# Two feed-forward layers behind an attention kernel: widening products by Strassen's algorithm in sets of seven, narrowing products in blocks behind them

## The reference

```python
scores = np.where(q_bucket == k_bucket, scale * q @ k.T, -1e9)
x = softmax(scores) @ v               # regrouped to x: 1536 x 512
h = sigmoid(x @ w_gate) * (x @ w_val) # widening, 512 -> 1536
x = h @ w_out                         # narrowing, 1536 -> 512
h = x @ w_in                          # widening, 512 -> 2048
g = where(h >= 1, h, where(h <= -1, 0, (h + 1)**2 / 4))
out = g @ w_out2                      # narrowing, 2048 -> 512
```

## Time and profile before

| | us |
|---|---|
| median of 3 runs | 810.24 (810.23 to 810.4) |
| the profiled execution | 812.36 |
| its span, first to last instruction | 810.3 |
| TensorE (PE) busy | 798.3 |
| its weight loads (PEld) | 687.4 |
| VectorE (DVE) busy | 377.4 |
| ScalarE (ACT) busy | 393.3 |
| GpSimd (POOL) busy | 241.6 |

### The profile page before, as it was taken

One profiled execution on the slowest core, in us unless ns is written; L12 is line 12 of the kernel. 1 busy time (PEld: TensorE's weight loads), 2 busy tenths in 40 slices (PEclk: granted clock), 3 DMA queues, 4 the chain that ended last, 5 costly groups with the idle time before them and its releaser, 6 DMA issues.

```text
span 810.3 us, 10651 instructions
## 1 busy us (share of the span) xinstructions
PE 798.3 (99%) x4015; PEld 687.4 (85%) x4015; DVE 377.4 (47%) x624; ACT 393.3 (49%) x636; POOL 241.6 (30%) x248
## 2 busy tenths in 40 slices
PE   7999999999999999999999999999999999999997
PEld 7899999999888888888888888888888888888886
DVE  5888888888793211131112221234434443344333
ACT  4889988988995332121112232335434333343332
POOL 4567767866865633000000043422100000000000
PEclk9999999999999999999999999999999999999999
DMA  6896586465302331000000023220000100010001
GB/s 140 175 204 139 125 171 140 89 138 122 101 1 74 122 114 55 1 1 1 0 1 1 0 78 105 79 78 27 1 0 1 53 1 0 1 53 0 1 1 52
DMA packets 62002, 49.51 MB, mean 61 GB/s; under 512 B 28592, under 2 KB 51840, under 8 KB 61824
## 3 DMA queue, kind: packets, MB, share of 16 engines
q1 hardware_dynamic: 61792, 48.83, 25.0%
q10 hardware_dynamic: 160, 0.00, 0.0%
HBM read 27.27 MB, written 3.15 MB: 38 GB/s over the span
## 4 chain that ended last, share of the span: by engine, by line
PE 90%; DVE 4%; ACT 3%; issue 2%; DMA 1%; POOL 0%; SPq 0%; ACTq 0%
PE ps L569 17%; PE ps L571 17%; PE ps L570 17%; PE ps L545 6%; PE ps L693 5%; PE ps L695 5%; PE ps L694 5%; PE ps L562 3%; PE ps L563 3%; PE ps L533 3%; PE ps L536 3%; DVE probs L952 2%; PE ps L496 2%; DVE body L963 1%; ACT body L733 1%
## 5 line engine op out<-in xcount | busy, mean ns | idle before, releaser
L569 PE MATMUL ps<-xh,arena 128*128 128x512 f32 x480 | 186.9, 389 | 0.0
L571 PE MATMUL ps<-xh,arena 128*128 128x512 f32 x480 | 186.8, 389 | 0.0
L570 PE MATMUL ps<-xl,arena 128*128 128x512 f32 x480 | 186.8, 389 | 0.0
L425 POOL TENSOR_TENSOR arena<-stage,arena 128x1024 fp32r<-128x1024 f32 (+1 forms) x26 | 73.4, 2831 | 253.5 <-ACT arena L763 253.5
L1022 DVE TENSOR_TENSOR gate<-ps,gate 128x512 f32<-128x512 f32 x36 | 24.9, 692 | 200.6 <-ACT gate L821 200.6
L821 ACT ACTIVATE gate<-ps 128x512 f32<-128x512 f32 x36 | 21.5, 598 | 176.9 <-PE ps L571 176.9
L963 DVE TENSOR_TENSOR body<-ps,body 128x768 fp32r<-128x768 f32 x96 | 91.7, 956 | 32.4 <-ACT body L733 31.2
L569 PEld LDWEIGHTS ps<-xh,arena 128*128 128x128 f32 x480 | 90.1, 188 | 18.9 <-issue 0.4
L571 PEld LDWEIGHTS ps<-xh,arena 128*128 128x128 f32 x480 | 90.1, 188 | 18.8
L570 PEld LDWEIGHTS ps<-xl,arena 128*128 128x128 f32 x480 | 90.1, 188 | 18.6
L418 POOL TENSOR_SCALAR probs<-probs,small 128x768 f32<-128x768 f32 x96 | 86.8, 913 | 25.5 <-DVE small L957 22.7
(11 more groups left out here) (95 smaller groups left out, 1194.0 us busy)
## 6 DMA issues: line engine op xcount, KB each, us to landing
stage<-in_moe_w_out_dram SPq DMA_DIRECT2D x28, 256.0 KB, 3.3
body<-qh SPq DMA_DIRECT2D x15, 384.0 KB, 5.3
body<-kh SPq DMA_DIRECT2D x28, 192.0 KB, 5.4
stage<-in_moe_w_in_dram SPq DMA_DIRECT2D x16, 256.0 KB, 2.8
qn<-in_q_dram SPq DMA_DIRECT2D x16, 192.0 KB, 4.6
kn<-in_k_dram SPq DMA_DIRECT2D x16, 192.0 KB, 5.8
body<-ql SPq DMA_DIRECT2D x16, 192.0 KB, 5.7
vn<-in_v_dram SPq DMA_DIRECT2D x16, 192.0 KB, 2.6
```

What stands on the lines that cost most here:

```text
L569: pe.matmul(dst, wh, ah, start=start, stop=False)
L570: pe.matmul(dst, wh, al, start=False, stop=False)
L571: return pe.matmul(dst, wl, ah, start=False, stop=stop)
```

## The change

The hidden features are now made in sets. A set takes 256 features (F) for one batch of 768 tokens, contraction 512, as a product of 2 x 2 blocks, and makes it with Strassen's algorithm (the form with 15 additions) from seven products instead of eight, each with 256 of contraction, 128 features and 384 tokens. There are 24 sets for the first layer (N1; gate and value in turns, six pairs for each batch) and 16 for the second (N2, "hinge"). FIRSTS are the sets 0, 12, 24, 32, where a new batch or layer begins.

The sums of the weight blocks (four of 256 elements a set) are made on POOL, as are the low parts (low_a: 512 and 256 elements, low_s: 1024), after ScalarE's round_w; only two sets of split weights are kept, and each batch makes them again. The four sums of the x blocks and the seven low parts are made on VectorE, 768 elements each (sum_x, rest_x), the high parts on ScalarE (round_x); for set 0 four sums are on POOL within the last attention steps. Products use PSUM banks 6 and 7 in turn (4 and 5 in sets 0 and 1). ScalarE copies out the first product of a set, VectorE adds the others to what it has (empty). In the first layer the value's set ends in gate_quarter (384 elements) and gate_tiles (768 and 384). A hidden tile is 128 features x 768 tokens; round_tile (ScalarE) and rest_tile (VectorE) split it. empty_y copies a finished narrowing result out of PSUM. In the narrowing of the first layer each block of 128 output features takes 768 tokens as 512 and 256 columns. Behind the seventh product of each set stands a block of narrowing work of earlier tiles (units, down): four units of six matmuls in the first layer, eight in set 24, twelve of three matmuls in the others. hinge_part is Relu and Square of 768 elements on ScalarE.

```diff
+    R = 7
+    F = 2 * P
+    N1, N2 = 2 * B * (T1 // 2), B * (T2 // 2)
+    NSETS = N1 + N2
+    FIRSTS = (0, N1 // 2, N1, N1 + N2 // 2)
+    PAIRS1 = N1 // 2
+    TILES1 = 2 * PAIRS1
...
+        LEFT = (0, 4, 1, 5, 3, 2, 6)
+        def bank(n, r):
+            q = R * n + r
+            return ps[:, (4 if n < 2 else 6) + q % 2, 0:G]
+        def emptied(n, r):
+            if r < 0:
+                n, r = n - 1, r + R
+            return (e_dve, (R - 1) * n + r) if r else (e_act, n + 1)
...
+            for n in range(2, NSETS):
+                sp.wait_ge(w_split, 2 * (n - 1))
+                load_w(n)
+                if 2 < n < N1 // 2 and n % 2:
+                    sp.wait_ge(wo_split, n // 2)
+                    load_wo(wo_v, n // 2)
+                if N1 <= n < FIRSTS[3]:
+                    sp.wait_ge(wo_split, T1 // 2 + n - N1)
+                    load_wo(wo2_v, n - N1)
...
-            def product(dst, wh, wl, ah, al, start, stop):
-                pe.matmul(dst, wh, ah, start=start, stop=False)
-                pe.matmul(dst, wh, al, start=False, stop=False)
-                return pe.matmul(dst, wl, ah, start=False, stop=stop)
-            def up1(g, f, which):
-                pe.wait_ge(w_split, f + 1)
-                if not (g == 0 and f < 2):
-                    pe.wait_ge(gated, T1 * g + f - 1)
-                for m in which:
-                    dst = ps[:, 4 + 2 * m + f % 2, :]
-                    for c in range(KT):
-                        if f == 0 and m == 0:
-                            pe.wait_ge(xh_ready, 2 * g + c // 2 + 1)
-                            pe.wait_ge(xl_ready, 2 * g + c // 2 + 1)
-                        at_w = 2 * C1 * f + DM * m + P * c
-                        last = product(dst, arena[:, at_w:at_w + P], arena[:, at_w + C1:at_w + C1 + P],
-                                       xh[:, c, :], xl[:, c, :], c == 0, c == KT - 1)
-                if 1 in which:
-                    last.then_inc(hid_ready, 1)
+            def product(n, r):
+                if r < 2:
+                    pe.wait_ge(w_split, 2 * n + r + 1)
+                if n in FIRSTS:
+                    pe.wait_ge(x_low, low_count(group_of(n), r))
+                if n == 2 and r == 0:
+                    pe.wait_ge(o_last, 3)
+                if R * n + r > 1:
+                    pe.wait_ge(*emptied(n, r - 2))
+                high, low = weights(n, 0)[:, LEFT[r]], weights(n, 1)[:, LEFT[r]]
+                dst = bank(n, r)
+                for c in range(2):
+                    pe.matmul(dst, high[:, c, :], high_x(r)[:, c, :], start=(c == 0), stop=False)
+                    pe.matmul(dst, high[:, c, :], low_x(r)[:, c, :], start=False, stop=False)
+                    last = pe.matmul(dst, low[:, c, :], high_x(r)[:, c, :], start=False, stop=(c == 1))
+                last.then_inc(p_done, 1)
...
+            def down1(t, c):
+                if c == 0:
+                    tile_waits(t)
+                wh, wl = narrow(t)
+                cols, first, last_tile = slice(P * c, P * c + P), t % T1 == 0, t % T1 == T1 - 1
+                main, rest = ps[:, c, :], ps[:, 4 + c // 2, (S - 512) * (c % 2):(S - 512) * (c % 2) + S - 512]
+                if first and c % 2 == 0:
+                    pe.wait_ge(zeroed, 1)
+                    pe.matmul(ps[:, 4 + c // 2, :].rearrange("p (a n) -> p a n", a=2), zero[:, :],
+                              hh[:, t % 3, 512:S].rearrange("p (a n) -> p a n", a=1).to_broadcast([P, 2, S - 512]),
+                              start=True, stop=False)
+                for n, (w, h) in enumerate(((wh, hh), (wh, hl), (wl, hh))):
+                    pe.matmul(main, w[:, cols], h[:, t % 3, 0:512], start=(first and n == 0), stop=(last_tile and n == 2))
+                    last = pe.matmul(rest, w[:, cols], h[:, t % 3, 512:S], start=False,
+                                     stop=(last_tile and n == 2 and c % 2 == 1))
...
+            def units(n, r):
+                if n < 2 or r < R - 1:
+                    return 0
+                return KT if n < N1 else 2 * KT if n == N1 else 2 * T
...
             pe.wait_ge(ends[held[2][0]], held[2][1] + 1)
-            up1(0, 0, (0,))
+            product(0, 0)
+            product(0, 1)
             turn_probs(STEPS - 3)
             turn_probs(STEPS - 2)
             for part in range(HT):
                 weigh(2 * NH - 2, part)
             turn_probs(STEPS - 1)
-            up1(0, 1, (0,))
+            product(0, 2)
+            product(0, 3)
             for part in range(HT):
                 weigh(2 * NH - 1, part)
-            pe.wait_ge(o_last, 2)
-            up1(0, 0, (1,))
-            pe.wait_ge(o_last, 3)
-            up1(0, 1, (1,))
+            for r in range(4, R):
+                product(0, r)
+            for n in range(1, NSETS):
+                for r in range(R):
+                    product(n, r)
+                    for _ in range(units(n, r)):
+                        down()
+            last2 = TILES1 + 2 * T2 - 2
+            for r in range(T):
+                down2(last2, r)
+            for r in range(T):
+                down2(last2 + 1, r)
...
+            def first_product(n):
+                act.wait_ge(p_done, R * n + 1)
+                if n:
+                    act.wait_ge(*emptied(n - 1, 2))
+                    if widens(n - 1) == "value":
+                        act.wait_ge(half_gated, pair_of(n - 1) + 1)
+                act.copy(u1[:, :], bank(n, 0)).then_inc(e_act, 1)
+            def sigmoids(n):
+                pp = pair_of(n)
+                for second in (1, 0):
+                    act.wait_ge(*emptied(n, 6 - second))
+                    act.activation(hidden(pp, second), hidden(pp, second), ACT.Sigmoid).then_inc(sig_done, 1)
...
+            def gate_set(n):
+                pp, after = pair_of(n), n in FIRSTS
+                g = group_of(n)
+                if n == FIRSTS[1] + 2:
+                    empty_y(0)
+                first_product(n)
+                round_tile(2 * pp - 2)
+                if after:
+                    round_x(g, 5)
+                    round_x(g, 6)
+                round_tile(2 * pp - 1)
+                round_w(n + 1)
+                sigmoids(n)
...
+            def hinge_set(n):
+                pp, g = pair_of(n), group_of(n)
+                t = 2 * pp
+                ahead = n + 1 in FIRSTS
+                first_product(n)
+                round_tile(t - 2)
+                if n in FIRSTS:
+                    round_x(g, 5)
+                    round_x(g, 6)
+                if t - 1 > TILES1:
+                    hinge_part(t - 1)
+                if ahead:
+                    round_x(g + 1, 0)
+                    round_x(g + 1, 1)
+                round_tile(t - 1)
+                if n + 1 < NSETS:
+                    round_w(n + 1)
+                if n < FIRSTS[3]:
+                    f = n - N1
+                    if f < T1 // 2:
+                        act.wait_ge(tile_used, TILES1 // 2 + 2 * f + 2)
+                    else:
+                        act.wait_ge(x_low, 3 * R)
+                    round_wo(T1 // 2 + f, (narrow2(2 * f), narrow2(2 * f + 1)))
+                if ahead:
+                    round_x(g + 1, 2)
+                    round_x(g + 1, 3)
+                hinge_part(t)
+                if ahead:
+                    round_x(g + 1, 4)
+                if n in (N1, FIRSTS[3]):
+                    empty_y(g - 1)
...
+            def empty(n, r):
+                pp = pair_of(n)
+                value = widens(n) == "value"
+                dve.wait_ge(p_done, R * n + r + 1)
+                one, two = hidden(pp, 0), tmp if value else hidden(pp, 1)
+                if r == 1:
+                    dve.wait_ge(*emptied(n, 0))
+                    if n:
+                        dve.wait_ge(*emptied(n - 1, 6))
+                        if widens(n - 1) == "value":
+                            dve.wait_ge(gated, 2 * pair_of(n - 1) + 2)
+                    dst, other = u2, u1
+                elif r == 2:
+                    if pp > 1 and not value:
+                        dve.wait_ge(hl_ready, 2 * (pp - 1))
+                    dst, other = u1 if value else one[:, 0:G], u1
+                elif r == 3:
+                    dve.wait_ge(*emptied(n, 1))
+                    dst, other = u3, u2
+                elif r == 4:
+                    dve.wait_ge(*emptied(n, 3))
+                    dve.tensor_tensor(two[:, G:S], bank(n, 4), u3, ALU.add)
+                    dst, other = u2, u2
+                elif r == 5:
+                    dst, other = two[:, 0:G], u3
+                else:
+                    dve.wait_ge(*emptied(n, 4))
+                    dst, other = u2 if value else one[:, G:S], u2
+                dve.tensor_tensor(dst, bank(n, r), other, ALU.add).then_inc(e_dve, 1)
+            def rest_tile(t):
+                dve.wait_ge(hh_ready, t + 1)
```

(102 more changed lines are left out.)

728 lines of the change are left out of this document (396 added, 332 removed).

## The result

The changed kernel takes 867.29 us (median of four runs) against 810.32 for the kernel before on the same chip: ratio 1.0707, 95% interval 1.0686 to 1.0728. The prediction had the direction, and VectorE as the engine that TensorE waits for, but its range ended at 866 (the bounds that it worked out itself went to 871). The profiled execution took 867.23 us for a span of 865.1; the forecast's sum, made against the span of before, was 810.3 + 32.8 = 843.1, so 22 us more than forecast are to be found, beside the 33 that were forecast.

A forecast was written before the change was run, and what follows sets the result against it. TensorE's matmul issue was taken to bound the kernel. Matmul list -26.9, set and border waits +16.7 and +40.8, bridge out of attention +3.3, removed waits -1.1: +32.8 on 810.2 gives 843 us, range 818 to 866.

The forecast's parts named there:

- the matmul list: Feed-forward matmuls on TensorE: Strassen's products and the 512 + 256 narrowing take 528.8 us against 555.7, 26.9 us less.
- the handshake: Products through two PSUM banks, each emptied before reuse: TensorE waits 16.7 us in stage one, 40.8 in stage two.
- P4: Fifth of a set's products P0 to P6: forecast to start 1.59 us late in a hinge set.
- P6: Seventh product of a set, waiting for P4's two reading instructions: forecast 0.35 us late in a hinge set.
- P5: Sixth product of a set: forecast not late in value sets, 0.32 us late in gate sets.
- the last attention steps: Bridge out of attention: TensorE waits 2.0 us for rests of x, 1.1 in set 0, 0.2 in set 1.
- At nothing. POOL: POOL's weight work, 7.4 us in a set of 12 to 17, ready in time and priced at no cost.
- Rival 2, the clock: Pauses in stage two lower the clock to the 1.2 GHz level: 97 us more, 940; chance 0.03.
- The sizes at the borders: Waits at group borders: sets 11, 23 2.9 us each; 12, 24 2.2; 25, 33 3.5; 31 6.2; 32 4.1.
- Rival 1: VectorE's empties keep up, leaving P6's wait, 13 us, and 5 us at borders: 800 us; chance 0.11.

The follow-up runs named there:

- the run with the order repaired and POOL light: Changed kernel with hinge tiles finished in their own set, ScalarE copying the fifth product, x's work spread, and POOL's weight work on 8 of 128 columns: 799.83 us.
- POOL light: Changed kernel with POOL making weight sums and low parts on 8 of 128 columns from set 2 on (output not right): 847.45 us.
- best complete kernel: Changed kernel with hinge tiles finished in their own set, x's work spread over sets, VectorE still emptying the fifth product, POOL's work whole: 831.21 us.

## Why the prediction was right about the direction and short on the size

**Right: the matmul list.** A pair of 512 and 256 columns takes 0.35 us; the next matmul starts 0.12 after one of 256 columns (forecast 0.125):

```profile
304.10 0.28 PE L760 MATMUL ps<-hh,wo 128*128 128x256 f32 x1
304.22 0.40 PE L759 MATMUL ps<-hl,wo 128*128 128x512 f32 x1
304.45 0.28 PE L760 MATMUL ps<-hl,wo 128*128 128x256 f32 x1
```

So the saving was there: the sets of 11.55 us in the run with the order repaired and POOL light have no wait in them (42 x 0.176 + 12 x 0.35 = 11.6). The Trainium skill's estimate of 37 us ("TensorE: Matmul & The Clock Gate", Back-to-back issue gap) would need 0.109 for 256 columns and 0.1625 for 384; the traces show 0.12 and 0.176, so the rows decided rightly. The page gives that formula for a matmul by itself; these stand in a stream with a weight load each.

**Right: the handshake.** In a regular hinge set of the changed kernel P4 starts 1.4 to 1.7 us late and P6 0.2 to 0.35; forecast 1.59 and 0.35. The reason given is the work between two empties: a rest and the hinge, which waits for ScalarE's Square. The run that moves it away shows it: 17.4 to 17.9 us become 15.8 to 15.9. The wait for ScalarE is the smaller part of it, 0.43 us in set 34 (the prediction's working has 0.37); the two instructions of 0.96 are the larger.

```profile
752.76 0.96 DVE L1270 TENSOR_TENSOR hid<-hid,tmp 128x768 f32<-128x768 f32 x1 [0.43 <-ACT tmp L958]
```

In the value sets the forecast had P5 on time; it is 0.33 late there with POOL whole and on time with POOL light. Beside and behind the last attention steps TensorE waits for rests of x three times, 2.7 us in all, for a forecast of 3.1.

**Wrong: the step "At nothing. POOL".** It asked only whether POOL's own chain is ready in time, and for TensorE it was. (By the prices that it gives, 1.28 us for 512 elements and 2.40 for 1024, its 7.4 us a set come to 6.9, and the low parts of the narrowing weights are not in them; the stretch of layer one has 9.4 in 12.1 us.) It left out what POOL does to others while it works. The failed term is therefore the duration of VectorE's instructions of 768 elements with both operands in SBUF: 0.98 in the sum, and 1.53 in the mean for x's rests and the gating, up to 3.1 us at the borders, in the changed kernel. What the runs show in its place: such an instruction that starts under one of POOL's ended 0.82 us after it, in the three cases above. The rows that I took it from the earlier trace rows are of a kernel in which POOL works 7% of the stretch; the change raises that to 78%. Four groups have that price: with 56 rests of tiles, 32 hinge adds, 27 rests of x and 12 gatings it is 56 x 0.05 + 32 x 0.16 + 27 x 0.55 + 12 x 0.54 = 29 us of VectorE's time over 0.98. The gates' additions of 384 elements (1.09 and 0.91 us for 0.55 and 0.57 with POOL light) and the sums of x add some 13 us over their durations with POOL light, and the clamps another 13. Of all this mostly what fell at the borders reached TensorE. The run with light POOL gives 20 us back.
The Trainium skill ("GPSIMD Engine Reference", 1. Specifications) says that GpSimd shares its SBUF interfaces with VectorE, with contention for instructions that take two inputs from SBUF or run in a 2-port mode. These traces agree on the first: with two SBUF inputs 693 ns become 916, while a reader of PSUM keeps 690 and 687. The clamp from one SBUF input goes from 560 to 973, which fits the second, though no run here shows the mode that it runs in. It was there to be read, and it spoke against this change.

**Rival 2, the clock,** was wrong in its form and not in its kind. The pauses of 1.3 to 1.6 us in each regular hinge set left the clock at 1.00. It fell to the 1.2 GHz level six times, for 3.4 us each, in sets 12, 24, 31 (twice), 32 and 33; P6 and the block of set 12 took 6.9 us in place of 5.4. The size of a pause alone doesn't tell: 0.6 and 1.5 us in set 33 were followed by a fall, 0.9 and 1.5 in set 25 were not. In part this is a second-hand cost of the same step: with POOL light the low level lasts 10.2 us in sets 31 and 33, for 20.5.

**The sizes at the borders** were otherwise fair: with POOL light, sets 11, 24, 25, 32 and 33 measure 14.4, 18.0, 18.7, 19.8 and 19.8 for a forecast of 14.5, 18.0, 19.1, 19.7 and 19.1; set 31 is 23.4 for 21.8, set 12 14.4 for 13.8.

**Rival 1** (the empties keep up, 800) did not hold. That the kernel with the order repaired and POOL light takes 799.8 is a coincidence of numbers: its waits were taken away by edits, not by a shorter round trip.

**Open:** the 1.9 us before set 0 are argued from the traces only. The same attention steps run 1.9 us earlier than in the kernel before until 204 us, and 1.9 us later at 237; in between POOL works on the first x, with five instructions of 1.5 to 2.5 us (201.94, 209.76, 217.29, 225.08 and 232.58) among the normalises that the steps wait for. The prediction put these at nothing too ("up to 1.8 us at a time", with slack). No run leaves them out. In the best complete kernel the borders remain. Spreading x's work over a whole group would need a second copy of its operands (7 x 2 x 2 x 384 x 4 bytes, 43 KB a partition); it was not tried. No complete version here beats the kernel before; only the one that leaves out most of POOL's work does.

## What to carry to other kernels

Saving matmuls makes TensorE a customer of the engines that feed and empty it; price their durations with the load that they will have after the change, not with that of the trace in hand. An engine whose own results are in time can still be the cost: look for instructions of VectorE with two operands in SBUF beside POOL's, and for others from SBUF that take longer beside it than alone. And when one repair gives little, try it together with the other before dropping either: two limits on one path can hide each other (20 and 27 us alone, 67 together here).

## What was not expected of the hardware

- POOL and VectorE don't share evenly. A VectorE instruction with two SBUF operands that starts under a POOL instruction of 1024 elements lasted until 0.82 us after it: 2.88 us for 0.95 of work at 390.25, 3.10 at 407.27. POOL pays too: its additions of 256 elements take 0.72 to 0.74 us alone and 1.44 beside VectorE (396.21 to 400.46), and its 1024-element rest goes from 2.37 to 3.06.
- A single-operand clamp from SBUF on 768 elements takes 0.56 us with POOL light and 0.97 with it at work, so it loses more than the additions do (0.97 to 1.14).
- Pauses of 1.3 us in every 17.5 never lowered the granted clock. Behind pauses of 1.05 and 3.60 us it fell, to the 1.2 GHz level from 411.7 to 415.1.
